# Attention and two mixture layers: scale and bias of a row in one operation, and x of the first batch turned through the last two heads

## What is computed

```python
q_bits = (np.einsum('bhsd,dk->bhsk', q, proj) > 0)      # the same for k
mask = q_bucket[:, :, :, None] == k_bucket[:, :, None, :]
scores = (1.0 / np.sqrt(D)) * np.matmul(q, k.transpose(0, 1, 3, 2))     # D = 64
scores = np.where(mask, scores, -1000000000.0)
scores = scores - np.max(scores, axis=-1, keepdims=True)
attn = np.exp(scores); attn = attn / (np.sum(attn, axis=-1, keepdims=True) + 1e-09)
out = np.matmul(attn, v)
x = out of all heads side by side, 1536 x 512
# dense mixture: P from the gates, then for each expert
out += P[:, e:e + 1] * (np.maximum(x @ w1[e], 0.0) @ w2[e])
# sparse mixture: x + gate * (relu(x @ w1[e]) @ w2[e]) for active tokens
```

## Time and profile before

| | us |
|---|---|
| median of 3 runs (1350.77, 1354.65, 1355.5) | 1354.65 |
| profiled execution | 1356.91 |
| its span, first to last instruction | 1355.1 |
| TensorE busy (matmuls) | 1318.6 (97%) |
| VectorE busy | 848.4 (63%) |
| ScalarE busy | 569.7 (42%) |
| GpSimd busy | 305.5 (23%) |

### The profile page before, as it was taken

The page is one execution under the profiler, slowest core; times in us unless marked ns, Lnnn a source line. Parts: engine busy times, 40 slices in busy tenths (PEclk is TensorE's granted clock), DMA queues, the critical chain, the costliest instruction groups (busy, mean ns, idle before and its releaser), DMA issues.

```text
span 1355.1 us, 24730 instructions
## 1 busy us (share of the span) xinstructions
PE 1318.6 (97%) x9435; PEld 763.7 (56%) x9435; DVE 848.4 (63%) x1491; ACT 569.7 (42%) x870; POOL 305.5 (23%) x229
## 2 busy tenths in 40 slices
PE   6999999899999999999999999999999999998987
PEld 3776767665455456445545644654564465556665
DVE  5999999786576247436634742753464275567983
ACT  5999999652134114304312420440242043226662
POOL 4787776522002100300300030030003000121211
PEclk9999999999999999999999999999999999998989
DMA  9345441051011011001101100200110112468940
GB/s 235 95 100 124 111 110 36 37 204 62 1 62 63 1 62 62 0 0 66 58 0 62 62 0 28 72 23 0 62 62 0 62 63 78 180 205 281 342 151 21
DMA packets 51631, 109.84 MB, mean 81 GB/s; under 512 B 5216, under 2 KB 8840, under 8 KB 51568
## 3 DMA queue, kind: packets, MB, share of 16 engines
q1 hardware_dynamic: 48880, 105.40, 24.6%
q0 software_dynamic: 2240, 3.35, 0.7%
q10 hardware_dynamic: 448, 0.19, 0.1%
HBM read 93.57 MB, written 17.34 MB: 82 GB/s over the span
## 4 chain that ended last, share of the span: by engine, by line
PE 89%; DVE 4%; ACT 3%; issue 2%; DMA 1%; SPq 1%; POOL 0%; ACTq 0%; POOLq 0%; DVEq 0%
PE ps L1696 14%; PE ps L1699 14%; PE ps L1700 14%; PE ps L1722 11%; PE ps L1724 11%; PE ps L1725 11%; PE ps L1617 5%; PE ps L1605 2%; PE ps L1607 2%; PE ps L1589 2%; PE ps L1627 1%; PE ps L1629 1%; PE ps L1631 1%; ACT probsT_hi L808 1%; ACT probs L801 1%
## 5 line engine op out<-in xcount | busy, mean ns | idle before, releaser
L1722 PE MATMUL ps<-x_hi,w_hi 128*128 128x384 f16 x896 | 292.3, 326 | 2.3 <-DVE parts L1275 1.2
L1724 PE MATMUL ps<-x_lo,w_hi 128*128 128x384 f16 x896 | 292.3, 326 | 0.0
L1725 PE MATMUL ps<-x_hi,w_lo 128*128 128x384 f16 x896 | 292.3, 326 | 0.0
L1699 PE MATMUL ps<-w_lo,h 128*128 128x512 f16 x768 | 291.2, 379 | 0.0
L1700 PE MATMUL ps<-w_hi,h 128*128 128x512 f16 x768 | 291.2, 379 | 0.0
L1696 PE MATMUL ps<-w_hi,h 128*128 128x512 f16 x768 | 291.1, 379 | 0.0
L1332 DVE SCALAR_TENSOR_TENSOR x<-ps,gate_now,x 128x512 f32<-128x512 f32 x84 | 63.1, 751 | 251.6 <-PE ps L1700 250.6
L938 ACT ACTIVATE x1s<-ps 128x384 f32<-128x384 f32 x64 | 30.4, 475 | 326.5 <-PE ps L1725 326.5
L636 POOL TENSOR_TENSOR wf<-wf 128x1024 f32<-128x1024 f32 x8 | 18.8, 2355 | 633.1 <-PE ps L1725 622.4
L955 ACT ACTIVATE h<-parts 128x1152 f16<-128x1152 f32 x64 | 74.4, 1163 | 140.2 <-DVE parts L1290 140.2
L1700 PEld LDWEIGHTS ps<-w_hi,h 128*128 128x128 f16 x768 | 75.1, 98 | 90.6
(11 more groups left out here) (229 smaller groups left out, 2270.3 us busy)
## 6 DMA issues: line engine op xcount, KB each, us to landing
wf<-w1a SPq DMA_DIRECT2D x32, 512.0 KB, 6.0
w_stage_in<-w2a SPq DMA_DIRECT2D x8, 2048.0 KB, 8.7
w_in<-w1b SPq DMA_DIRECT2D x4, 2048.0 KB, 9.5
w_in<-w2b SPq DMA_DIRECT2D x4, 2048.0 KB, 9.8
w_in_b<-w1b SPq DMA_DIRECT2D x4, 2048.0 KB, 10.0
w_in_b<-w2b SPq DMA_DIRECT2D x4, 2048.0 KB, 10.2
rows<-blank SPq DMA_DIRECT2D x1, 6682.0 KB, 21.5
qk_in<-kT SPq DMA_DIRECT2D x32, 192.0 KB, 4.3
```

The costliest lines, as they stand in the source:

```text
L1699: pe.matmul(acc, a_hi, b_lo, start=False, stop=False)
L1722: pe.matmul(group_bank(g, role), w_hi, x_hi, start=(opens and kt == 0), stop=False, skip_group_check=not opens)
L1724: pe.matmul(group_bank(g, role), w_hi, x_lo, start=False, stop=False, skip_group_check=not opens)
L1725: last = pe.matmul(group_bank(g, role), w_lo, x_hi, start=False, stop=(kt == 1), skip_group_check=not opens)
```

## The change

Seven edits, which belong together in parts.

1. `take_max`: the maximum is stored negated beside a constant one in `row_top`, and one operation makes scale and bias of the row: (negated maximum < threshold) times the pair (1, negated maximum).
2. The factor 1/8 of the scores, which was in the scale, is put into the casts of queries and keys, as a scale for each partition (`qk_scale`) read from SBUF; five memsets on VectorE prepare it and the constant one.
3. x of the first batch is turned one tile at a time in steps 0, 2, 3, 4, 5 and 6 of the last pair, and ScalarE takes all of its tiles.
4. GpSimd casts and subtracts the blocks 0, 4 and 6 of x itself; ScalarE and VectorE do the four sums. VectorE makes two of the four low parts in the last two steps of attention, the other two behind them.
5. The normalisation of head 14 moves between GpSimd's sums of x.
6. GpSimd's scalings of values and of the first expert's weights take the factor as a constant (`tensor_scalar`), where they read it from SBUF as a second tensor.
7. The last two tiles of x of the second batch are turned after the second product of group 1, not after the fifth.

```diff
-X_HI = (0, 4, 6, 2, 1, 3, 5)
-X_LO_DVE, X_LO_POOL = (1, 2, 3, 5), (0, 4, 6)
-TAKEN_BY_DVE = (1, 3, 4, 5)
+X_SUMS, X_BLOCKS = (2, 1, 3, 5), (0, 4, 6)
+TURNED_AT = (0, 2, 3, 4, 5, 6)
...
-                scale = v_scale[:, :].unsqueeze(1).to_broadcast([P, QT, D])
-                pool.tensor_tensor(V_hi[r][:, :, 0:D], V_in[r][:, :, :], scale, ALU.mult
+                pool.tensor_scalar(V_hi[r][:, :, 0:D], V_in[r][:, :, :], V_SCALE, 1.0, ALU.mult, ALU.mult
...
-                pool.tensor_tensor(w7_hi[:, k, :, :], wf[:, k, :, :], scale, ALU.mult).then_inc(w1_hi_ready, 1)
+                pool.tensor_scalar(w7_hi[:, k, :, :], wf[:, k, :, :], W_SCALE, 1.0, ALU.mult, ALU.mult
+                                   ).then_inc(w1_hi_ready, 1)
...
+            def split_x_block(b, k):
+
+                n = len(X_BLOCKS) * b + X_BLOCKS.index(k) + 1
+                pool.wait_ge(xf_ready, QT * b + (QT if k == 6 else QT // 2))
+                pool.tensor_scalar(x7_hi[:, b, k, :, :], x_block(k, b), 1.0, 1.0, ALU.mult, ALU.mult
+                                   ).then_inc(x7_hi_pool, 1)
+                pool.wait_ge(x7_hi_pool, n)
                 pool.tensor_tensor(x7_lo[:, b, k, :, :], x_block(k, b), x7_hi[:, b, k, :, :], ALU.subtract
                                    ).then_inc(x7_lo_pool, 1)
...
-                act.activation(A[r][:, 1, :], qk_in[r][:, 1, :], ACT.Copy).then_inc(qk_hi, 1)
+                act.activation(A[r][:, 1, :], qk_in[r][:, 1, :], ACT.Copy, scale=qk_scale[:, 1:2]).then_inc(qk_hi, 1)
...
-                act.activation(probs[r][:, :], psS[r], ACT.Exp, bias=row_bias[:, slot:slot + 1],
-                               scale=row_scale[:, slot:slot + 1]).then_inc(probs_ready, 1)
+                act.activation(probs[r][:, :], psS[r], ACT.Exp, bias=row_scale_bias[:, slot, 1:2],
+                               scale=row_scale_bias[:, slot, 0:1]).then_inc(probs_ready, 1)
...
-                    if last and s >= QT:
-                        first_x(s - QT)
+                    if last and s in TURNED_AT:
+                        take_xf(TURNED_AT.index(s))
+                    if last and s >= 2 * QT - 4:
+                        x7_hi_part(0, s - 2 * QT + 4)
...
-                dve.tensor_reduce(row_max[:, slot:slot + 1], psS[r], AX.X, ALU.max
+                dve.tensor_reduce(row_top[:, slot, 1:2], psS[r], AX.X, ALU.max, negate=True
                                   ).then_inc(max_ready, 1)
                 between()
 
                 dve.wait_ge(max_ready, i + 1)
-                dve.tensor_scalar(row_scale[:, slot:slot + 1], row_max[:, slot:slot + 1],
-                                  -0.5 * Q_MASK * K_MASK, EXP_SCALE, ALU.is_gt, ALU.mult
-                                  ).then_inc(scale_ready, 1)
-                dve.wait_ge(scale_ready, i + 1)
-                dve.tensor_scalar(row_bias[:, slot:slot + 1], row_max[:, slot:slot + 1],
-                                  row_scale[:, slot:slot + 1], -1.0, ALU.mult, ALU.mult
-                                  ).then_inc(bias_ready, 1)
+                dve.scalar_tensor_tensor(out=row_scale_bias[:, slot, :],
+                                         in0=row_top[:, slot, 1:2].to_broadcast([P, 2]),
+                                         scalar=0.5 * Q_MASK * K_MASK, in1=row_top[:, slot, :],
+                                         op0=ALU.is_lt, op1=ALU.mult).then_inc(bias_ready, 1)
...
-                    if last and s in (QT + 1, QT + 2, QT + 3):
-                        take_xf((1, 3, 5)[s - QT - 1])
...
-                    if last and s == QT + 2:
-                        take_xf(4)
+                    if last and s >= 2 * QT - 2:
+                        x7_lo_part(0, X_SUMS[s - 2 * QT + 2])
...
-                    if turns_x:
-                        turn_x(2 * (s - QT))
+                    if last and s in TURNED_AT:
+                        turn_x(TURNED_AT.index(s))
...
                     group_product(g, 1, 4, 1, True)
+                    if first and g == 1:
+                        turn_x(QT + 4)
+                        turn_x(QT + 5)
```

More of the change, by code:

```diff
@@ L348, in x_tile @@
             return xf[:, t // QT, :, (t % QT) * P:(t % QT + 1) * P]
-        def act_tiles(t):
-            return sum(u not in TAKEN_BY_DVE for u in range(t + 1))
-        def dve_tiles(t):
-            return sum(u in TAKEN_BY_DVE for u in range(t + 1))
-        def x_hi_count(b, k):
-            return NP * b + X_HI.index(k) + 1
         def group_bank(g, role):
@@ L683, in _ @@
                 split_first_w1(j - 1)
-            normalise(G - 2)
             pool.wait_ge(v_split, 3 * G)
@@ L713, in sum_and_split_x @@
             def sum_and_split_x(b):
-                x7_lo_part(b, 0)
-                x7_lo_part(b, 4)
+                split_x_block(b, 0)
+                if b == 0:
+                    split_x_block(b, 4)
                 sum_x(b)
-                x7_lo_part(b, 6)
+                if b > 0:
+                    split_x_block(b, 4)
+                split_x_block(b, 6)
             for b in range(B):
@@ L792, in split_k @@
                 reached(act, scores_done, QT * g - QT)
-                act.activation(A[r][:, 1, :], qk_in[r][:, 1, :], ACT.Copy).then_inc(qk_hi, 1)
+                act.activation(A[r][:, 1, :], qk_in[r][:, 1, :], ACT.Copy, scale=qk_scale[:, 1:2]).then_inc(qk_hi, 1)
             def split_q(r):
-                act.activation(A[r][:, 0, :], qk_in[r][:, 0, :], ACT.Copy).then_inc(qk_hi, 1)
+                act.activation(A[r][:, 0, :], qk_in[r][:, 0, :], ACT.Copy, scale=qk_scale[:, 0:1]).then_inc(qk_hi, 1)
             def exp(i, slot, r):
@@ L831, in _ @@
             act.dma_start(const[:, 0:P], consts[:, 0:P]).then_inc(consts_in, 16)
+            act.wait_ge(scales_set, 5)
             act.wait_ge(first_k, 32)
-            act.activation(A[0][:, 1, :], qk_in[0][:, 1, :], ACT.Copy).then_inc(qk_hi, 1)
+            act.activation(A[0][:, 1, :], qk_in[0][:, 1, :], ACT.Copy, scale=qk_scale[:, 1:2]).then_inc(qk_hi, 1)
             act.wait_ge(first_q, 32)
@@ L844, in take_xf, with x7_hi_part @@
                                scale=X_SCALE).then_inc(xf_ready, 1)
-            def x7_hi_part(b, k):
-                if k in (0, 4, 6):
-                    last_tile = QT * b + (QT - 1 if k == 6 else QT // 2 - 1)
-                    act.wait_ge(xf_ready, act_tiles(last_tile))
-                    act.wait_ge(xf_dve, dve_tiles(last_tile))
-                else:
-                    act.wait_ge(sums_pool, 4 * b + {2: 1, 1: 2, 3: 3, 5: 4}[k])
-                act.activation(x7_hi[:, b, k, :, :], x_block(k, b), ACT.Copy).then_inc(x7_hi_ready, 1)
-            def first_x(step):
-                if step in (0, 1):
-                    take_xf(2 * step)
-                if step in (1, 2, 4, 5):
-                    x7_hi_part(0, X_HI[(1, 2, 4, 5).index(step)])
+            def x7_hi_part(b, n):
+                act.wait_ge(sums_pool, len(X_SUMS) * b + n + 1)
+                act.activation(x7_hi[:, b, X_SUMS[n], :, :], x_block(X_SUMS[n], b), ACT.Copy).then_inc(x7_hi_ready, 1)
             def pair(j, first, last):
@@ L905, in w2_part @@
                 w2_hi_part(c, w2_stage_in, w2_hi, W_SCALE, (w2_loaded, 16 * e + 16), w2_hi_ready)
-            for k in X_HI[QT - 2:]:
-                x7_hi_part(0, k)
             def second_x(g, place):
@@ L1083, in _ @@
         def _(dve):
+            for half, of_q, of_k in ((slice(0, 64), EXP_SCALE, 1.0), (slice(64, P), 1.0, EXP_SCALE)):
+                dve.memset(qk_scale[half, 0:1], of_q).then_inc(scales_set, 1)
+                dve.memset(qk_scale[half, 1:2], of_k).then_inc(scales_set, 1)
+            dve.memset(row_top[:, :, 0:1], 1.0).then_inc(scales_set, 1)
             dve.memset(least[:, :], 0.0).then_inc(least_ready, 1)
@@ L1186, in _ @@
             take_probsT_lo(NTILES - 1, 1, 1)
-            def x7_lo_part(b, k):
-                dve.wait_ge(x7_hi_ready, x_hi_count(b, k))
-                dve.tensor_tensor(x7_lo[:, b, k, :, :], x_block(k, b), x7_hi[:, b, k, :, :], ALU.subtract
-                                  ).then_inc(x7_lo_dve, 1)
-            for k in X_LO_DVE:
+            for k in X_SUMS[2:]:
                 x7_lo_part(0, k)
@@ L1300, in expert @@
                     if first and g in (2, 3):
-                        for k in X_LO_DVE[2 * (g - 2):2 * (g - 1)]:
+                        for k in X_SUMS[2 * (g - 2):2 * (g - 1)]:
                             x7_lo_part(1, k)
@@ L1650, in turn_x @@
                     pe.wait_ge(x_ready, G // 2)
+                    pe.wait_ge(qk_lo, 2 * G)
                 elif t < QT:
-                    pe.wait_ge(*((xf_dve, dve_tiles(t - 1)) if t - 1 in TAKEN_BY_DVE else (xf_ready, act_tiles(t - 1))))
+                    pe.wait_ge(xf_ready, t)
                 elif t == QT:
@@ L1667, in pair @@
                     g, r, q = 2 * j + s // QT, s // QT, s % QT
-                    turns_x = last and QT <= s < QT + 3
```

(6 more changed lines are left out.)

62 lines of the change are left out of this document (28 added, 34 removed).

## The result

The changed kernel takes 1369.68 us (median of 4 runs, 1366.61 to 1373.63), the kernel before on the same chip 1355.08 (4 runs). The ratio is 1.0112, 95% interval 1.0094 to 1.013: **14.6 us slower**. The profiled execution has a span of 1366.9 us against 1355.1, at a granted clock of 0.996. In this kernel the operation that makes scale and bias is line 1102, the maximum 1097, the low parts of the turned exponentials 1091, the exponential 796, GpSimd's low parts of keys and queries 575 and 581.

The account below looks back on a forecast made before the run. In attention three engines are nearly full, VectorE near the bound but not it; its waits for GpSimd would make it so. 20 + 0.2 + 0.3 + 0.7 = +21 us on 1354.65: 1375.7 us, range 1352 to 1392.

Parts of the forecast that it names:

- The step on which everything hung: Attention tiles: each of the 96 new two-element VectorE operations waits for whatever instruction GpSimd is in the middle of.
- The first rival: Scale-and-bias operation doesn't wait; pointer casts and x alone give +2.8 us, 1357.5 us; chance 0.24.
- the second, faster: VectorE sets the pace of a pair of heads, so 0.19 us less per tile passes on: 1340 us; chance 0.08.
- the two-input rule: A VectorE instruction with two SBUF inputs and a GpSimd instruction reading SBUF contend; the second is blocked throughout the first.
- 0.48 us: Mean wait of each new operation for GpSimd, from squared durations over twice the period; 5.8 us for 12 tiles.
- The low and high bounds, 0.25 and 0.82: Wait in us if most arrivals find a gap (nothing lost), or always meet a half-done 1.64 us operation (+48 us).
- 31.5 us: Pair of heads with VectorE as the bound: work 24.7, waits 5.8, plus waits for ScalarE; before 28.7.
- I had added 1.0: VectorE's remaining wait for ScalarE behind the two casts, 0.5 us a head, added to the pair of heads.
- +20 us: Loss over the seven pairs of heads with loads, at 2.8 us a pair, from VectorE's waits for GpSimd.
- The pointer was counted as hidden: Casts with scale from SBUF: 0.09 us each, counted as nothing in the heads behind a VectorE that is the bound.
- +0.3 and +0.7: us for turning x through the last two heads (between -1.5 and +2), and for the late turn in the second dense group.
- the -1.15: TensorE's wait of 1.15 us at 255.59 goes, because two differences of x are made before the last head ends.

Follow-up runs that it names:

- e2: Changed kernel, still one two-element scale-and-bias operation, but its pair lies in PSUM and the other tensor input is an SBUF constant: 1359.35 us, ratio 1.0032.
- e5: Kernel before plus only the new scale-and-bias operation and the casts with scale by pointer; x and GpSimd's long scalings kept: 1367.28 us, ratio 1.0094.
- e3: Changed kernel with a one-element mask operation, then a two-element operation with a single SBUF tensor input multiplying the pair by it: 1378.57 us, ratio 1.018.
- e4: Changed kernel with GpSimd's long scalings back, reading the factor as a second tensor: 1373.1 us, ratio 1.0137.
- e6: e2 without the pointers of the query and key casts, so the score factor is left out: 1357.57 us, ratio 1.0018.
- e9: e7 without the pointers of the casts, so the score factor is left out: 1355.77 us, ratio 1.0008.
- e10: Changed kernel without the pointers of the casts, so the score factor is left out: 1367.08 us, ratio 1.0096.
- e7: e2 with x turned and taken as in the kernel before: 1356.97 us, ratio 1.0015.
- e1: Changed kernel with its one scale-and-bias operation turned back into two one-element operations, all else kept: 1362.4 us, ratio 1.0053.

## Why the prediction was right, and where its sizes were off

**The step on which everything hung was right.** The two-element operation waits for GpSimd's running instruction to its end (125.07 and 135.10 above); e2 takes the wait away and 10.9 us with it, e5 puts it, with the pointers, into the kernel before and loses 12.7. The spread is 0.16 to 1.62 us, VectorE's share rises though it does less, TensorE's wait moves to VectorE's low parts. The first rival, no wait, is refuted, and so is the second, faster: with the wait gone, one operation in place of two brings 0.13 us a pair and not 12 x 0.19. The prediction called the cast of 12 elements a case of the two-input rule; it has one input, so that at a small size only a one-input operation had been seen. The changed kernel shows the wait at two elements with two inputs, and e3 with one.

**The wait was sized at 0.48 us and is 0.41.** The sum of squares used 1.31 and 0.49 us for GpSimd's scalings; they take 1.05 and 0.51 to 0.57. With these, and 0.89 and 0.83 us measured for the other operations on values, it is (4 x 2.69 + 2 x 0.97 + 2 x 0.79 + 2 x 0.69 + 4.56 + 4/7 x 5.5 + 2 x 1.10 + 2 x 0.32 + 2 x 0.26) / (2 x 30.1) = 26.7 / 60.2 = 0.44 us. The low and high bounds, 0.25 and 0.82, did not come about. That arrivals at a random moment describe it so well is in part luck: for e4 the same sum gives 0.51 us, and the trace has 0.40.

**The pair was forecast at 31.5 us and takes 30.1.** The new operation without a wait takes 0.16 us, not the 0.21 taken from the old bias: VectorE's work in a pair is 24.7 - 12 x 0.05 = 24.1. With 12 x 0.41 = 4.9 of waits that is 29.0, and VectorE is idle for 204.30 - 196.44 = 7.9 us in about seven pairs, 1.1 in each, where I had added 1.0. The sum is 30.1. It has to come out, since the idle time is read from the result; what it tests is the 1.0, which was a guess and a good one. Both mis-sized terms, the wait and the work, erred the same way: +20 us was +10.2 from start to last cast of keys. That the total came within 6 us is in part luck, because the pointer and x, below, were counted too low.

**The pointer was counted as hidden, and is hidden by half or more.** Its size, 0.09 us for each cast, was right. Where VectorE doesn't wait it costs 0.37 us a pair (e6, e9), more than the 0.24 of the first rival; in the changed kernel at most 0.20 (e10), where I had nothing. The Trainium skill, "ScalarE: Activation LUTs", section "What ACT_TABLE_LOAD costs", gives about 93 ns for each pointer operand; the trace agrees for the scale of a copy, 936 - 844 = 92 ns. The +0.2 us before the first exponential can't be checked: the fourth cast of keys comes at 41.0 to 43.6 us in the thirteen profiles, in no order that the pointer explains.

**x was forecast at +0.3 and +0.7 and costs more.** The steps take 2.83 us, as said (242.28 to 245.11). The last part was 3.6 - 2.1 = 1.5 in my sum; it measures 1.7 where the new operation doesn't wait (e2 against e7, e6 against e9), 2.0 in e4 against e5, and 2.5 in the changed kernel, in which waits of line 1102 are part of it. What failed is the -1.15: the wait at the first low part did go, but others came in its place: in e2 the wait for VectorE's parts grew by 1.37, because the low parts of the second batch met GpSimd, and the changed kernel waits 0.60 + 0.53 us for ScalarE's copy of line 918. The late turn costs TensorE 0.52 us (276.26), not 0.7. e2 against e7 gives 4.3 - 2.0 = +2.3 us for all edits of x, with overlapping intervals, against +1.0 forecast; that is inside the bound of +2 for the first part and 0.7 for the second.

**The dense part came out 0.9 us shorter**, where +0.7 was forecast less 1.15. Near the end the changed kernel was granted a higher clock. By stretches, the changed kernel:

```profile
1200.00:1240.00 40.00, 35.09 (x330) 21.57 (x328) 26.31 (x89) 12.37 (x18) 10.27 (x11) 0.99 0.64 207
```

and the kernel before:

```profile
1200.00:1240.00 40.00, 34.99 (x347) 24.83 (x345) 28.72 (x81) 14.80 (x21) 7.64 (x9) 0.91 0.77 265
```

The clock is 0.99 in the one and 0.91 in the other. The dense parts of the table differ by 5.5 us between kernels that do nearly the same there, so nothing is built on 0.9.

**What is not closed.** e1 has two operations that never wait, yet its pair of heads takes 29.04 us, 0.25 more than e2 and 0.12 more than the kernel before with the pointer's 0.37. e2's advantage over it suggests that VectorE's own work is not quite free, but the 0.12 has no cause here. By the ratios e1 is 7.2 us behind the kernel before; the pointers (7 x 0.37 = 2.6) and x (2.3) explain 4.9 of them, and of the rest a part may be the 3.4 us at the lower clock in its last part. No version beats the kernel before: e9, which leaves out the factor, only equals it.

## What to carry to other kernels

Before an operation on VectorE is merged or widened, look at whether it gets two inputs in SBUF, or goes from SBUF to SBUF on more than one element, and whether GpSimd is busy beside it. A two-element operation could then take 1.6 us in place of 0.16; operations on one element of one tensor, and the one with its pair in PSUM, ran through. And ask first whether the engine that is relieved sets the pace: here 14 us less work on VectorE brought 0.13 us a pair, and nothing that the whole time shows.

## What the runs showed of the hardware that was not expected

- A `tensor_scalar` with one SBUF input waits for GpSimd at two elements (228 to 1706 ns) and never at one (153 to 156 ns), e3.
- `scalar_tensor_tensor` on two elements takes 160 ns from SBUF without a wait and 221 ns with one operand and the scalar in PSUM, and there it varies by 3 ns beside a busy GpSimd (e2).
- GpSimd's product by a constant takes 1047 ns for 1024 elements and 513 for 384 (changed kernel), where the product of two tensors takes 1893 and 827 (e4).
- An operation that begins in the last 0.13 us of GpSimd's instruction doesn't wait any more: it takes 0.16 us at 91.67, where GpSimd's ends at 91.79 (e4).
- The mean wait doesn't fix the cost: 563 ns on average made pairs of 30.41 us in e4, 569 ns pairs of 30.10 in the changed kernel. Why is open.
